# An inverse of 128 triangular blocks: VectorE alone, or VectorE on half-sized blocks with TensorE joining them

## The reference

```python
for t in range(S):                                  # per batch and head, state is 40 x 40
    y[t] = r[t] @ state
    Sa = state @ a[t]
    state = state * w[t][None, :] - outer(Sa, b[t]) + outer(v[t], k[t])
# first MLP, 320 -> 2048 -> 320
h = x @ w_in;  x = (h - tanh(h)) @ w_out
# four experts, 320 -> 1024 -> 320, weighted by normalised probabilities
out = sum_e p[:, e] * (relu(x @ w1[e]) @ w2[e])
```

## Time and profile before

| | us |
|---|---|
| median of 3 runs | 1586.53 |
| lowest, highest | 1586.33, 1588.02 |
| the profiled execution | 1586.63 |
| span of the profiled execution | 1584.8 |
| mean granted TensorE clock | 0.978 |

### The profile page before, as it was taken

The page is one execution under the profiler, slowest core; times in us unless marked ns, Lnnn a source line. Parts: engine busy times, 40 slices in busy tenths (PEclk is TensorE's granted clock), DMA queues, the critical chain, the costliest instruction groups (busy, mean ns, idle before and its releaser), DMA issues.

```text
span 1584.8 us, 37837 instructions
## 1 busy us (share of the span) xinstructions
PE 1461.1 (92%) x15888; PEld 1276.6 (81%) x15888; DVE 829.0 (52%) x1457; ACT 399.1 (25%) x814; POOL 367.3 (23%) x313
## 2 busy tenths in 40 slices
PE   3378789999999999999969999999999999999998
PEld 2266668878878977977958889999999999999997
DVE  7979768777777876944113343233323332333233
ACT  1022333333333333333323221111111111111111
POOL 6121545333332332312325302010020202020000
PEclk9977899999999999999989999999999999999999
DMA  8454683165066054030030320001010101000011
GB/s 220 132 145 117 183 210 102 45 169 135 5 184 155 6 155 123 1 85 24 1 108 1 90 67 29 8 0 36 0 37 0 36 0 36 0 0 0 0 50 50
DMA packets 87671, 108.71 MB, mean 69 GB/s; under 512 B 13630, under 2 KB 66686, under 8 KB 87542
## 3 DMA queue, kind: packets, MB, share of 16 engines
q1 hardware_dynamic: 86190, 106.17, 24.9%
q10 hardware_dynamic: 1352, 0.66, 0.2%
HBM read 75.94 MB, written 30.84 MB: 67 GB/s over the span
## 4 chain that ended last, share of the span: by engine, by line
PE 81%; DVE 11%; DMA 2%; issue 1%; POOL 1%; ACT 1%; SPq 1%; POOLq 0%; DVEq 0%; ACTq 0%
PE banks L1575 22%; PE banks L1585 21%; PE banks L875 10%; PE banks L884 9%; PE banks L644 2%; DVE tmp L1136 2%; DVE ld L1133 2%; PE banks L759 2%; DVE nvmak L1193 2%; PE banks L724 2%; PE banks L707 2%; PE banks L716 1%; PE banks L737 1%; PE banks L763 1%; PE banks L617 1%
## 5 line engine op out<-in xcount | busy, mean ns | idle before, releaser
L1575 PE MATMUL banks<-x2t,u 128*128 (+1 forms) x1536 | 376.7, 392 | 0.0
L1585 PE MATMUL banks<-u,hid 128*128 128x320 f32 x2304 | 362.5, 309 | 0.0
L1585 PEld LDWEIGHTS banks<-u,hid 128*128 128x128 f32 x2304 | 349.9, 188 | 13.1 <-issue 0.9
L1679 DVE SCALAR_TENSOR_TENSOR hid<-banks,hid 128x512 fp32r<-128x512 f32 x192 | 132.8, 692 | 404.5 <-ACT hid L1665 404.5
L1575 PEld LDWEIGHTS banks<-x2t,u 128*128 128x128 f32 x1536 | 282.4, 188 | 52.7
L1665 ACT ACTIVATE hid<-banks 128x512 fp32r<-128x512 f32 x192 | 114.9, 598 | 564.8 <-PE banks L1575 564.8
L875 PE MATMUL banks<-xt,wi 128*128 128x512 f32 x768 | 195.4, 398 | 14.6 <-POOL xt L1362 13.6
L884 PE MATMUL banks<-wo,hid 128*128 128x320 f32 x1152 | 183.5, 310 | 2.0 <-POOL hid L1367 1.6
L884 PEld LDWEIGHTS banks<-wo,hid 128*128 128x128 f32 x1152 | 174.5, 188 | 10.8 <-POOL hid L1367 3.8
L875 PEld LDWEIGHTS banks<-xt,wi 128*128 128x128 f32 x768 | 141.1, 190 | 43.3 <-POOL xt L1362 13.9
L1367 POOL TENSOR_TENSOR hid<-shared,hid 128x512 fp32r<-128x512 f32 x96 | 124.4, 1296 | 210.6 <-ACT hid L1048 210.6
(11 more groups left out here) (117 smaller groups left out, 1513.9 us busy)
## 6 DMA issues: line engine op xcount, KB each, us to landing
scaled_operands<-made SPq DMA_DIRECT2D x79, 192.4 KB
kb<-scaled_operands SPq DMA_DIRECT2D x46, 192.0 KB
made<-kbaw SPq DMA_DIRECT2D x38, 192.0 KB
made<-kbaw SPq DMA_DIRECT2D x41, 144.0 KB
raw<-w SPq DMA_DIRECT2D x8, 640.0 KB, 5.8
lam<-scaled_operands SPq DMA_DIRECT2D x46, 96.8 KB
at<-scaled_operands SPq DMA_DIRECT2D x46, 96.0 KB
raw<-w SPq DMA_DIRECT2D x8, 512.0 KB, 4.0
```

The source lines that it names most:

```text
L1575: mm = pe.matmul(self.p_up[f][:], self.u1[:, par, w, f * 128:(f + 1) * 128], self.xt[:, bass.ds(n, 1), x, :].rearrange("p o t -> p (o t)") ...
L1585: mm = pe.matmul(self.p_dn[t][:, 0:D], self.hid[:, f, h, t * 128:(t + 1) * 128], self.u2[:, par, w, f, :], start=(f == 0 and i == 0), stop ...
L1679: dve.scalar_tensor_tensor(out=ex.hid[:, f, 1, :], in0=ex.p_up[f][:], scalar=0.0, in1=ex.hid[:, f, 0, :].bitcast(F32), op0=ALU.max, op1=AL ...
```

## The change

In the first two chunks the inverse of a 32x32 block is made from its quarters. VectorE inverts the two 16x16 diagonal quarters, both in the same instructions, in 15 columns instead of 31. TensorE computes the lower left quarter as two products for each block: first the off-diagonal quarter times one inverse (`cross_products`), saved by ScalarE (`save_cross`), then that times the other inverse (`corner_products`); VectorE adds it into `tt`. Each of the two steps is 128 matmul calls (32 blocks of four heads) with 16 or 32 rows and 16 columns. The 66 steps become 40 for these chunks. `inverse_end` and `inverse_begin` count them. The numbers of interleaved steps in pairs 1 to 3 go down; the last four, two of them after a wait for TensorE, come behind pair 3. Chunks 2 to 5 keep the old inverse.

```diff
+SUB = BLK // 2
+ALONE = 7 + 2 * (SUB - 1)
+JOINED = ALONE + 2
+HALVED = 2
...
+    upright = sb("upright", [128, SUB, BLK])
...
+    folded = gap.rearrange("p a t -> p (a t)")
+    lower = folded.rearrange("p (a i k) -> p a i k", a=2, k=BLK)[:, :, :, 0:SUB]
+    solved = folded.rearrange("p (a i k) -> p a i k", a=2, k=BLK)[:, :, :, SUB:BLK]
+    cross = folded[:, 0:SUB * BLK]
...
             if b == 0 and j == 0 and p % PPC == 0:
-                pe.wait_ge(inv_step, (p // PPC + 1) * INV_STEPS)
+                pe.wait_ge(inv_step, inverse_end(p // PPC))
...
+        def cross_products(c):
+
+            if c:
+                for j in range(2):
+                    pe.wait_ge(un_saved[j], NB * PPC * c)
+            pe.wait_ge(inv_step, inverse_begin(c) + ALONE - 1)
+            for m in range(BLK):
+                for h in range(GH):
+                    part = slice(BLK * h, BLK * h + SUB)
+                    mm = pe.matmul(answer_bank[block_of(h), m * SUB:(m + 1) * SUB], ld[part, m, :], upright[part, :, m],
+                                   start=True, stop=True)
+            mm.then_inc(cross_full, 1)
+
+        def corner_products(c):
+
+            pe.wait_ge(cross_saved, c + 1)
+            pe.wait_ge(inv_step, inverse_begin(c) + JOINED)
+            for m in range(BLK):
+                for h in range(GH):
+                    part = slice(BLK * h, BLK * h + SUB)
+                    mm = pe.matmul(turn_bank[part, m * SUB:(m + 1) * SUB], cross[block_of(h), m * SUB:(m + 1) * SUB],
+                                   tt[block_of(h), SUB:BLK, m], start=True, stop=True)
+            mm.then_inc(corner_full, 1)
...
+            joins = p % PPC == 0 and p < HALVED * PPC
+            if joins:
+                cross_products(p // PPC)
             for i in prepared[:1]:
                 diagonal(i)
             if p and not after_mlp:
                 scores_ur(p - 1)
+            if joins:
+                corner_products(p // PPC)
             answer(p, 0, 0)
...
+        def save_cross(c):
+            act.wait_ge(cross_full, c + 1)
+            act.wait_ge(inv_step, inverse_begin(c) + ALONE + 1)
+            act.activation(cross, answer_bank, ACT.Copy).then_inc(cross_saved, 1)
...
+        def halved_inverse(c, first, last):
+
+            base = inverse_begin(c)
+            for k in range(first, last):
+                if k:
+                    dve.wait_ge(inv_step, base + k)
+                if k == 0:
+                    dve.wait_ge(lt_saved, (c + 1) * NG)
+                    dve.wait_ge(op_stored[RING + 1], 32)
+                    ins = dve.transpose(folded[:, 0:SUB * BLK].rearrange("p (t k) -> p t k", k=BLK),
+                                        ld[:, :, 0:SUB].rearrange("p m t -> p t m"))
+                elif k == 1:
+                    ins = dve.transpose(folded[:, SUB * BLK - SUB:BLK * BLK - SUB].rearrange("p (t k) -> p t k", k=BLK),
+                                        ld[:, :, SUB:BLK].rearrange("p m t -> p t m"))
+                elif k == 2:
+                    ins = dve.memset(solved, 0.0)
+                elif k == 3:
+                    ins = dve.memset(folded.rearrange("p (a x) -> p a x", a=2)[:, :, SUB::BLK + 1], -1.0)
+                elif k < 4 + 2 * (SUB - 1):
+                    j, sub = divmod(k - 4, 2)
+                    nr, ncol = SUB - 1 - j, j + 1
+                    t = tmp[:, 0:2 * nr * ncol].rearrange("p (a i k) -> p a i k", a=2, i=nr)
+                    if sub:
+                        ins = dve.tensor_tensor(out=solved[:, :, j + 1:, 0:ncol], in0=solved[:, :, j + 1:, 0:ncol], in1=t,
+                                                op=ALU.subtract)
+                    else:
+                        ins = dve.tensor_tensor(out=t, in0=bc(lower[:, :, j + 1:, j:j + 1], [128, 2, nr, ncol]),
+                                                in1=bc(solved[:, :, j:j + 1, 0:ncol], [128, 2, nr, ncol]), op=ALU.mult)
+                elif k == ALONE - 3:
+                    ins = dve.memset(lower, 0.0)
+                elif k == ALONE - 2:
+                    ins = dve.transpose(upright[:, :, :], folded.rearrange("p (i k) -> p k i", k=BLK)[:, SUB:BLK, :])
+                elif k == ALONE - 1:
+                    dve.wait_ge(smb_full[1], NB * PPC * c)
+                    ins = dve.transpose(tt[:, 0:SUB, :],
+                                        folded[:, SUB:SUB + SUB * BLK].rearrange("p (i k) -> p i k", k=BLK))
+                elif k == ALONE:
+                    ins = dve.transpose(tt[:, SUB:BLK, :], folded[:, SUB * BLK:BLK * BLK].rearrange("p (i k) -> p i k", k=BLK))
+                elif k == ALONE + 1:
+                    dve.wait_ge(kbn_saved[1], PPC * c + 1)
+                    if c:
+                        dve.wait_ge(ut_saved, PPC * c)
+                    ins = dve.memset(turn_bank, 0.0)
+                else:
+                    dve.wait_ge(corner_full, c + 1)
+                    corner = tt[:, SUB:BLK, :]
+                    ins = dve.tensor_tensor(out=corner, in0=corner,
+                                            in1=turn_bank.rearrange("p (m i) -> p i m", i=SUB), op=ALU.add)
+                ins.then_inc(inv_step, 1)
...
-            steps = {1: (0, 0, 0, 0, 8), 2: (6, 6, 6, 4, 6), 3: (6, 6, 6, 4, 6)}.get(p, (0, 0, 0, 0, 0))
+            steps = {1: (0, 0, 0, 0, 4), 2: (4, 4, 4, 2, 4), 3: (4, 4, 3, 2, 1)}.get(p, (0, 0, 0, 0, 0))
```

More of the change, by code:

```diff
@@ L80, in uses, with inverse_end, inverse_begin @@
     return sum(slot(k) == slot(i) for k in range(i + 1))
+def inverse_end(c):
+    return HALVED * (JOINED + 1) + (c + 1 - HALVED) * INV_STEPS if c >= HALVED else (c + 1) * (JOINED + 1)
+def inverse_begin(c):
+    return inverse_end(c - 1) if c else 0
 def prepared_in(p):
@@ L329, in recurrence_and_first_mlp @@
     inv_step = sem("inverse_step")
+    cross_full, cross_saved, corner_full = sem("cross_full"), sem("cross_saved"), sem("corner_full")
     def two(name):
@@ L938, in save_diagonal @@
             if c:
-                act.wait_ge(inv_step, c * INV_STEPS)
+                act.wait_ge(inv_step, inverse_end(c - 1))
             act.activation(ld[:, NB * g:NB * (g + 1), :],
@@ L1007, in start @@
             for i in range(8, FIRST):
+                if i == NG:
+                    save_cross(0)
                 save_diagonal(i)
@@ L1011, in pair @@
             prepared = [] if p and drained(p - 1) else first_diagonals(p)
+            if p == PPC:
+                save_cross(1)
             for i in prepared[:1]:
@@ L1108, in inverse @@
         def inverse(c, first, last):
-            base = c * INV_STEPS
+            base = inverse_begin(c)
             ti = ld
-            lu = gap.rearrange("p a (b t) -> p (a b) t", t=BLK) if c == 1 else tt
+            lu = tt
             for k in range(first, last):
@@ L1139, in inverse @@
                     dve.wait_ge(inv_step, base + k)
-                    if c == 1:
-                        dve.wait_ge(smb_full[1], NB * PPC * c)
                     ins = dve.transpose(tt[:, :, :], ti[:, :, :])
+                ins.then_inc(inv_step, 1)
+        def halved_inverse(c, first, last):
+            base = inverse_begin(c)
+            for k in range(first, last):
[28 more added lines that the diff above has]
+                elif k == ALONE - 1:
+                    dve.wait_ge(smb_full[1], NB * PPC * c)
+                    ins = dve.transpose(tt[:, 0:SUB, :],
[12 more added lines that the diff above has]
+                                            in1=turn_bank.rearrange("p (m i) -> p i m", i=SUB), op=ALU.add)
@@ L1148, in inverse_steps @@
             done = inverse_done.get(c, 0)
-            last = min(done + n, INV_STEPS)
-            inverse(c, done, last)
+            last = min(done + n, inverse_end(c) - inverse_begin(c))
+            if c < HALVED:
+                halved_inverse(c, done, last)
+            else:
+                inverse(c, done, last)
             inverse_done[c] = last
```

## The result

The changed kernel takes 1595.1 us against 1588.02 for the kernel before (medians of 19 runs each). The ratio of the two kernels is 1.0048, with a 95% interval of 1.0040 to 1.0057 (ratios here are taken over all runs of both kernels and need not equal the quotient of the medians): slower, and by more than the 0.2% that counts as no change. The forecast was 1580.1 us. The profiled execution has a span of 1593.7 us against 1584.8, 8.9 us more.

A forecast was written before the change was run, and what follows sets the result against it. TensorE, 92% busy, bounds the kernel on average, but chunk 0's VectorE inverse is pure path. Chunk, interleaved-step and clock terms sum to 24.4 - 4b; bursts of 17.9 us leave 6.5 off 1586.63: 1580.1 us, range 1574.5 to 1595.

The forecast's parts named there:

- The price of a burst: TensorE's 256 records per product step, four times in all, priced from the diagonal block's 32 records: 17.9 us together.
- b: Time of one TensorE burst of 256 records: 4.85 us taken for chunk 0's two, 4.1 for chunk 1's.
- 24.4 - 4b: Whole kernel's gain in us, all terms of chunks 0 and 1 less four bursts: 6.5 us.
- 53.25: Chunk 0: time in us when TensorE may start its first product, 13.55 us after VectorE's first transpose at 39.70.
- A cost between the bursts: Chunk 1's end: the next diagonal (0.39 us) and scores (1.1 us) standing between its two bursts on TensorE.
- VectorE's part: Chunk 0: VectorE's shortened inverse lets TensorE start 13.55 us in; the old inverse took 28.0 us.
- Pair 1's tail: End of pair 1: four new interleaved VectorE steps take 3.2 us where eight took 4.6, gain 1.4 us.
- Pair 2: Fewer interleaved VectorE steps in pair 2: gain 0.2 us in its middle and 3.1 at its end.
- Pair 3, up to the low scores saved: Pair 3: 13 interleaved VectorE steps instead of 22, 19.8 us instead of 22.05, gain 2.2 (0 to 5.1).
- The clock terms: TensorE holding its higher clock: gain 1.8 us in pair 4 and 0.5 in pairs 2 and 3.
- The slower case: In the four bursts, the moving operand's stride of 32 words slows records to 34 ns: 11 us slower, 1598; chance 0.24.
- The floor of 20 to 26 ns a record: In the bursts, records start no closer than this: gain 3.2 to -3.2 us, no change; chance 0.16.

The follow-up runs named there:

- Experiments 4: Changed kernel with only chunk 0 halved, same buffer, chunk 1 keeping the old inverse: 1592.24 us against 1587.48 for the kernel before, ratio 1.0026.
- experiment 6: Changed kernel with only chunk 0 halved, working in the buffer that is free earlier, chunk 1 old: 1587.13 us against 1585.21 for the kernel before, ratio 1.0009.
- Experiment 3: Changed kernel with moving operands read packed instead of at a stride of 32 words, values wrong: 1597.77 us against 1587.48 for the kernel before, ratio 1.0068.
- experiment 1: Changed kernel with chunk 0 in slot 5's buffer instead of slot 6's, free earlier: 1592.75 us against 1587.48 for the kernel before, ratio 1.0033.
- experiment 7: Kernel before plus 256 calls on constants, 16 moving columns, while TensorE waits for chunk 0's inverse: 1587.61 us, one run, against 1585.21.
- experiment 8: Kernel before plus 256 calls on constants, 128 moving columns, while TensorE waits for chunk 0's inverse: 1587.45 us, one run.

## Why the prediction was wrong

**The price of a burst failed.** The step was "the nearest row is the diagonal block", 18.1 or 12.2 ns a record, b = 4.85 or 3.3. As a rate while TensorE runs, that was high if anything: 14.5 ns for the first product and 9.8 for the second at the 2.4 GHz level. The levels came the other way round than assumed: chunk 0's bursts, costed at the lower one, ran at a granted clock of 1.00, and chunk 1's, costed between the two, fell to 0.50 behind the stop of 3.75 us. For the second product that changed nothing: its 128 records took 1.25 us at either level, as the busy time by stretch shows.

```profile
66.90:68.20 1.30, 1.24 (x128) 1.13 (x128) 0.00 (x0) 0.00 (x0) 0.00 (x0) 1.00 0.07 13
...
169.70:171.10 1.40, 1.25 (x128) 1.14 (x128) 0.00 (x0) 0.00 (x0) 0.00 (x0) 0.50 0.37 101
```

What failed is the step from 32 records to 256. The diagonal is shorter than what lies ready, so its row shows the rate of the engine and cannot show the rate of supply. From its first record to the next step's start a burst took 6.1 and 7.0 us in chunk 0 (57.77 to 63.83, 64.48 to 71.48), and 6.9 and 6.3 in chunk 1 (156.88 to ScalarE's save at 163.82, 168.09 to 174.38): 26.3 us in place of 17.9. With the prediction's own 24.4 - 4b that is a loss of 1.9 instead of a gain of 6.5. It had said that the sum turns at b = 6.1 us, and "that one price decides"; it did turn the sign, with 8.4 of the 15.6 us between forecast and trace. The rest are the terms that follow.

**A term was missing.** "53.25" for TensorE's first product rested on a first transpose at 39.70. But chunk 0's inverse now works in the buffer of a store, and `dve.wait_ge(op_stored[RING + 1], 32)`, which the old code had for chunk 1 alone, stands ahead of it: 4.65 us. The diff shows the line moved into the branch for both chunks; the prediction spoke of the changed semaphore counts as "other addresses and constants". The prediction put it at nothing. Experiments 4 and 6 differ in this and show 4.1 us of it at pair 0.

**A cost between the bursts.** The diagonal and the scores that stand between chunk 1's bursts were put at 0.39 + 1.1 us; they took 4.4 (163.71 to 168.09), with a stop of 1.49 among the diagonal's records. The granted clock of the records on either side of them was 0.50, the 1.2 GHz level, behind the stop of 3.75 us. That is 2.9 more.

**What was right.** VectorE's part: forecast 13.55 us (its terms add up to 13.6 to 13.7), measured 44.35 to 57.77, 13.4. Pair 1's tail: forecast 1.4, and the shift fell from 4.7 to 3.3 us. Pair 2: forecast 0.2 + 3.1, measured 3.8. Pair 3, up to the low scores saved: forecast 2.2 within 0 to 5.1, measured 22.05 - 18.0 = 4.05. In all 9.3 against 6.9. ScalarE's save did not come late because of its weight pieces (the last ends at 159.28, the save starts at 163.82). And time lost by pair 4 was still lost at the end.

**The clock terms** brought nothing that can be told apart: pair 4 took 18.4 us at 0.79 against 18.5 at 0.78, where 1.8 was forecast. In pairs 2 and 3 the granted clock did rise, from 0.79 and 0.73 to 0.83 and 0.91, and what that gave is inside the 9.3 us above. They had the thinnest rows under them.

The sum again with what was measured: 24.4 - 26.3 = -1.9; the wait -4.65; the steps between -2.9; the interleaved steps +2.4; the clock terms -2.2: -9.2 us. The trace says -9.1 at pair 4 and -8.9 at the end. That the sum closes this well is in part luck, since small terms left out of it cancel: chunk 0's other steps took 0.4 us less than costed, and pair 0 itself became 0.3 us longer.

**The rivals.** The slower case (0.24) had its end at 1598 through a strided operand, at b = 8.9. Experiment 3 refutes the stride: 2.79 us for 193 records either way. That the time came near 1598 all the same is luck: the bursts cost 6.6 us on the average, not 8.9, and the rest came from the wait and from the steps between. Instructions that do not arrive fast enough, a remark beside that rival, is what the runs show; it was given no price of its own, though TensorE's code is written out and the count of 512 instructions a burst stood in the text. The floor of 20 to 26 ns a record did not show: 9.8 ns. The rule of 25 ns between starts that the Trainium skill states (TensorE: Matmul & The Clock Gate, "Wait — 56ns, not 53.3ns?") does not hold in this trace for four heads' products in turn, although a burst with its stops comes to nearly the same on the average (26.3 / 4 = 6.6 us for 256, 25.7 ns), by another mechanism. The penalty for accesses that cross 16-byte lines, which the Trainium skill states (SBUF — State Buffer, "Door 1: The DMA port swizzle"), did not show on the moving operand in experiment 3.

What stays open: why one block takes 3.7 us at one time and 4.7 at another. The packets say where the time goes: from a block's first record to the start of the next packet it took 2.26 and 1.53 us in experiment 1 (blocks of 4.7 and 4.3 us), 1.60 and 1.12 in the changed kernel (4.2 and 3.7), 1.04 and 1.09 in experiment 6 (3.9 and 3.7); the packet itself took 1.1 to 1.4 us and TensorE started 1.2 to 1.5 us after it. What delays the start is not shown. In experiment 1 the DMA engines were 0.61 and 0.59 busy over these blocks, in the changed kernel 0.58 and 0.02, but in experiment 6 0.54 in one of 3.7 us: traffic alone doesn't order them.

## What to carry to other kernels

Count the instructions of a burst before its columns. Where TensorE's code is written out call by call, as here, and a product is shorter than the 28 to 37 ns at which records came here, the price of a burst is its count of instructions divided by the rate at which they come, less what lies ready at the start; a rate read from 32 records says nothing of 256. Pack more work into each call, even with half of the result thrown away, and let waits that are needed anyway stand where the next block has to come. And when code moves onto a path that had no wait, ask for each of its buffers who used it last.

## What the runs showed of the hardware

- TensorE's instructions came in blocks of 128 matmul records with their weight loads (256 instructions, one 16 KB packet of q8), 3.6 to 4.7 us apart, with nothing to wait for but them. Each stop ended 1.2 to 1.7 us after such a packet had landed, and after a stop the next packet started 1.0 to 2.3 us after TensorE had gone on. After waits of 12 to 16 us only 193 records lay ready (the 65 left of a block and one block more), so an idle engine does not gather more ahead.
- Records of fp32 products with 16 moving columns, four heads in turn, took 9.8 ns each on 32 rows with 16 stationary columns and 14.5 ns on 16 rows with 32 stationary columns, at a granted clock of 1.00 in both cases; the first kind took 9.8 ns at 0.50 too. On 32 rows with 32 stationary columns it was 14.8 ns with 16 moving columns (experiment 7) and 27 ns with 128 (experiment 8, behind a slower start).
- A moving operand at a stride of 32 words streamed as fast as a packed one: 193 records in 2.79 us for both.
- Keeping the wanted half of a double product cost VectorE two operations of 0.48 us on 128x256 out of PSUM, 0.5 us more between the bursts than ScalarE's plain save of 128x512.
